# Attention and two MLPs on one core: pair 1's loads held back behind pair 0's k, v loaded by one queue, and softmax sums read out of PSUM ahead of two weight tiles

## What is computed

```python
batch, n_heads, seq, head_dim = (2, 12, 448, 64)
scores = scale * np.matmul(q, k.transpose(0, 1, 3, 2))
scores = cap * np.tanh(scores / cap)
scores = scores - np.max(scores, axis=-1, keepdims=True)
attn = np.exp(scores)
attn = attn / (np.sum(attn, axis=-1, keepdims=True) + 1e-09)
attn_out = np.matmul(attn, v)                 # 2 x 12 x 448 x 64
x = attn_out.transpose(0, 2, 1, 3).reshape(896, 768)
h = x @ w_in1                                 # 768 x 2048
x = np.maximum(h, 0.0) ** 2 @ w_out1          # 2048 x 768
h = x @ w_in2
out = h * (1.0 / (1.0 + np.exp(-h))) @ w_out2
```

## Time and profile before

| | us |
|---|---|
| median of 3 runs | 546.67 |
| lowest, highest | 546.26, 548.05 |
| the profiled execution, its time | 548.26 |
| the profiled execution, its span | 546.5 |
| PE busy in the span | 536.2 |
| DVE busy | 376.6 |
| ACT busy | 261.1 |
| POOL busy | 82.2 |

### The profile page before, as it was taken

How to read it: one execution, slowest core, us unless ns; L and a number is a source line. 1 busy time by engine, 2 the same in 40 slices (tenths; PEclk the granted TensorE clock), 3 DMA queues, 4 the chain that set the end, 5 groups by cost and what they waited for, 6 DMA issues and landing times.

```text
span 546.5 us, 7023 instructions
## 1 busy us (share of the span) xinstructions
PE 536.2 (98%) x2620; PEld 441.9 (81%) x2620; DVE 376.6 (69%) x597; ACT 261.1 (48%) x403; POOL 82.2 (15%) x54
## 2 busy tenths in 40 slices
PE   7999999999999999999999999999999999999996
PEld 5333333799999999999998999999999999999995
DVE  3199999877778552776789855556865345568985
ACT  3998998054444322445444434544533244454230
POOL 0899999300000000000000000000000000000000
PEclk9999999999999999999999999999999999999999
DMA  8885530151202202410211114102111241020646
GB/s 228 211 222 154 150 107 17 42 136 58 56 22 76 59 1 58 136 58 23 56 52 43 42 59 135 58 5 74 38 49 48 59 122 44 29 78 3 125 66 89
DMA packets 82117, 42.17 MB, mean 77 GB/s; under 512 B 26784, under 2 KB 79008, under 8 KB 82080
## 3 DMA queue, kind: packets, MB, share of 16 engines
q1 hardware_dynamic: 77664, 40.12, 28.0%
q10 hardware_dynamic: 4384, 1.57, 1.2%
q0 software_dynamic: 32, 0.00, 0.0%
HBM read 38.93 MB, written 2.75 MB: 76 GB/s over the span
## 4 chain that ended last, share of the span: by engine, by line
PE 80%; DVE 13%; issue 3%; ACT 1%; DMA 1%; ACTq 0%; DVEq 0%
PE banks L501 26%; PE banks L503 26%; PE banks L502 26%; DVE den L829 3%; PE banks L443 2%; DVE x_hi L838 1%; DVE rinv L833 1%; DMA qk_raw<-in_q_dram 1%; DVE att_o L836 1%; DVE den_r L826 1%; DVE w_hl L879 1%; DVE qk_f L814 1%; PE banks L432 1%; DVE qk_f L810 1%; DVE y L959 1%
## 5 line engine op out<-in xcount | busy, mean ns | idle before, releaser
L501 PE MATMUL banks<-x_hi,w_hl 128*128 128x448 f32 x384 | 140.7, 366 | 0.0
L503 PE MATMUL banks<-x_hi,w_hl 128*128 128x448 f32 x384 | 140.5, 366 | 0.0
L502 PE MATMUL banks<-x_lo,w_hl 128*128 128x448 f32 x384 | 140.5, 366 | 0.0
L501 PE MATMUL banks<-g_hi,w_hl 128*128 128x448 f32 x336 | 123.4, 367 | 0.2 <-DVE w_hl L879 0.2
L503 PE MATMUL banks<-g_hi,w_hl 128*128 128x448 f32 x336 | 123.2, 367 | 0.0
L502 PE MATMUL banks<-g_lo,w_hl 128*128 128x448 f32 x336 | 123.2, 367 | 0.0
L501 PEld LDWEIGHTS banks<-x_hi,w_hl 128*128 128x128 f32 x384 | 72.1, 188 | 7.6 <-issue 1.4
L503 PEld LDWEIGHTS banks<-x_hi,w_hl 128*128 128x128 f32 x384 | 72.1, 188 | 6.2
L502 PEld LDWEIGHTS banks<-x_lo,w_hl 128*128 128x128 f32 x384 | 72.1, 188 | 6.2
L874 DVE TENSOR_TENSOR w_hl<-w_raw,w_hl 128x768 fp32r<-128x768 f32 x32 | 32.5, 1016 | 57.5 <-ACT w_hl L650 57.4
L682 ACT ACTIVATE work<-banks 128x448 f32<-128x448 f32 x64 | 31.3, 541 | 78.2 <-PE banks L503 69.2
(11 more groups left out here) (64 smaller groups left out, 549.7 us busy)
## 6 DMA issues: line engine op xcount, KB each, us to landing
w_raw<-in_moe_w_in_dram SPq DMA_DIRECT2D x32, 384.0 KB, 3.4
w_raw<-in_moe_w_out_dram SPq DMA_DIRECT2D x24, 512.0 KB, 5.2
qk_raw<-in_k_dram SPq DMA_DIRECT2D x44, 112.0 KB, 2.5
qk_raw<-in_q_dram SPq DMA_DIRECT2D x44, 112.0 KB, 2.7
out_dram<-rows SPq DMA_DIRECT2D x40, 56.0 KB, 2.2
v_t<-in_v_dram SPq DMA_DIRECT2D x22, 96.0 KB, 2.7
qk_raw<-in_k_dram ACTq DMA_DIRECT2D x4, 112.0 KB, 4.2
qk_raw<-in_q_dram ACTq DMA_DIRECT2D x4, 112.0 KB, 5.7
```

Of the source, the lines that this page charges most:

```text
L501: pe.matmul(dst, hi[:, kk, :], mov_hi, start=start, stop=False, skip_group_check=onto)
L502: pe.matmul(dst, hi[:, kk, :], mov_lo, start=False, stop=False, skip_group_check=onto)
L503: return pe.matmul(dst, lo[:, kk, :], mov_hi, start=False, stop=stop, skip_group_check=onto)
```

## The change

In three parts. SP and ACT each wait, after their four DMAs of pair 0, until k of pair 0 has landed, and only then issue those of pair 1. All four v DMAs of the first two pairs are issued by SP, none by ACT. `finish` is cut in two: `take_sums` waits for PE's sums and transposes them out of PSUM, `finish` does the rest; in the slots the two follow each other as before, and at the hand-over `take_sums` comes ahead of the weight tile's low part.

```diff
-            def load_v(part, groups=range(C)):
+            def load_v(part):
 
                 first, last = V_PARTS[part], V_PARTS[part + 1]
-                for g in groups:
+                for g in range(C):
@@ SP
             load_head(0, 0, k_v, 0, s_first_in[0])
             load_head(0, 1, q_v, 0, s_first_in[1])
+            sp.wait_ge(s_first_in[0], 4 * DMA)
             load_head(1, 0, k_v, 0, s_qk_in[1])
             load_head(1, 1, q_v, 0, s_qk_in[1])
-            load_v(0, range(0, 2))
+            load_v(0)
             load_v_x(0)
@@ ACT
             load_head(0, 0, k_v, 1, s_first_in[0])
             load_head(0, 1, q_v, 1, s_first_in[1])
+            act.wait_ge(s_first_in[0], 4 * DMA)
             load_head(1, 0, k_v, 1, s_qk_in[1])
             load_head(1, 1, q_v, 1, s_qk_in[1])
-            for g in range(2, C):
-                at = g * CW * D
-                act.dma_start(v_t[BL * g:BL * g + BL, 0:2 * V_PARTS[1], :],
-                              v_main[:, 0:2 * V_PARTS[1], at:at + CW * D]).then_inc(s_v_in[0], DMA)
@@ DVE
-            def finish(j, den_bank):
+            def take_sums(j, den_bank):
 
                 dve.wait_ge(s_att, j.no + 1)
                 dve.transpose(den_r[:, :], den_bank).then_inc(s_den, 1)
+
+            def finish(j):
+
                 dve.wait_ge(s_den, 4 * j.no + 1)
@@ DVE, slot(j)
-                finish(j + -2, den_ps(j + -2))
+                take_sums(j + -2, den_ps(j + -2))
+                finish(j + -2)
@@ DVE, hand-over
-            tile_low(0, 0, 0)
-            finish(At(0, PAIRS - 3), den_ps(At(0, PAIRS - 3)))
-            tile_low(0, 0, 1)
-            for j in range(PAIRS - 2, PAIRS):
-                finish(At(0, j), den_ps(At(0, j)))
+            for j in range(PAIRS - 3, PAIRS):
+                take_sums(At(0, j), den_ps(At(0, j)))
+                if j < PAIRS - 1:
+                    tile_low(0, 0, j - (PAIRS - 3))
+                finish(At(0, j))
```

## The result

The changed kernel took 545.39 us (median of 6 runs, 545.13 to 545.6), the kernel before 547.19 us (6 runs, 546.26 to 548.63): a ratio of 0.9961 with a 95% interval of 0.9949 to 0.9973, so 1.5 to 2.8 us less. A second set, with other runs of the kernel before beside it, gave 0.9963 (0.995 to 0.9977). The forecast was 1.4 us less and 545.3 us. The gain is about 2 us or 0.4%, just over what a measurement of this kernel can tell from no change.

What follows compares the result with a forecast made beforehand. PE was taken as full from 104 us on, so only its earlier arrival saves time: 0.77 us at the start plus 0.63 us at the hand-over, 546.67 - 1.4 = 545.3 us, range 544.5 to 546.6.

Steps and rivals of the forecast that it cites:

- Where time can be saved: From 104 us on PE is full, so the change helps only by letting PE get there earlier.
- Change 2: Hand-over before the MLPs: transposing pair 9's sums before tile_low lets PE's next sums start 0.6 to 0.66 us earlier.
- an unbroken sequence starts 0.08 us before the modelled end: Hand-over: PE's sums of pair 10 would start at 93.48, its values ending at 93.56, 0.66 us earlier.
- The tight spot: Near 102 us, PE's product waiting for the second tile_low: only 0.15 us left after the release.
- rival 4: Hand-over: tile_low(1) holds PE up, or sums aren't the wait; gain there 0 to 0.3 us, chance 0.13.
- Change 1: Start: holding pair 1's loads until pair 0's k lands frees q, so PE's first scores come 0.77 us earlier.
- the upper bound: Start: if cap's DMA lands earlier too, first scores gain up to 1.0 us, limited by PE's warm-up.
- pair 1 costs nothing: Start: pair 1's delayed loads land at 8.8 to 10.7, transposed by 12.0 at the latest, the limit; no cost.
- What lands behind SP's queue: First 28 us: v and the loads of pairs 2 and 3, issued later on SP, still arrive in time; no cost.
- rivals 2 and 3: SP's queue late: PE stands 0.85 us at 19 us, 546.1, chance 0.10; v late: 547.6 us, chance 0.05.
- The sum: Whole kernel: 0.77 us at the start plus 0.63 us at the hand-over makes 1.4 us, all reaching the end.
- the front: The kernel's start up to PE's first scores and values: 0.77 us expected gain, bounds 0 and 1.0.

Runs made afterwards that it cites:

- late_wait: Changed kernel, but both queues hold pair 1's loads until q of pair 0, not k, has landed: 548.63 us, ratio 1.0020.
- the front alone: Kernel before with only the wait for k and v's loads on SP, old hand-over kept: 546.68 us, ratio 0.9985.
- the hand-over alone: Kernel before with only the new hand-over, sums taken out of PSUM first, loads as before: 546.14 us, ratio 0.9978.
- sp_waits: Changed kernel, but only SP waits for k; ACT issues its half of pair 1 at once: 546.70 us, ratio 0.9988.
- act_waits: Changed kernel, but only ACT waits for k; SP issues its half of pair 1 at once: 548.59 us, ratio 1.0005.
- half_wait_w10: Changed kernel, pair 1 held only until each queue's first k DMA has landed, 10 warm-up matmuls for 14: 545.36 us, ratio 0.9965.

## Why the prediction held, step by step

- **Where time can be saved.** Held. Behind the hand-over the two programs run alike but for about 1 us that comes and goes with the execution.
- **Change 2, 0.63 us.** The right mechanism, undersized by a quarter: 0.80 to 0.85 us. The term "an unbroken sequence starts 0.08 us before the modelled end" was too small: the sums start 0.75 us behind the last four values, so 0.17 us before their end at 0.92, which gives 0.76. The other 0.05 is in the sums themselves, after which the next matmul now comes at 0.85 and not 0.90 us. The tight spot (rival 4, 0.15 us) never came up: I had left tile_low at 1.89 us, and it took 1.33 and 1.32 in its new place (the last section says why), the second ending at 100.14 with PE at its product at 100.95.
- **Change 1, 0.77 us.** The right mechanism, too large by about 0.3 us: 0.98 us between the first two profiles, 0.5 on average over three pairs. q was freed: without the waits it was late again. cap's DMA came earlier too, as the upper bound had allowed, so PE's warm-up became the limit at the first scores, which came at 7.93 on average and not at 8.15. The step that failed is "pair 1 costs nothing". My last landing was 8.8 to 10.7 and the limit 12.0 for the transposes; they ended at 11.93 and 12.26 (turned from 10.76 and 11.09), so the slack I had counted on was not there. Its price was small: from first scores to first values it is 4.99 to 5.00 us in the three traces with the old loads and 5.08 to 5.20 in those with the new, 0.1 to 0.2 us. `late_wait` shows how near the edge is. The larger error was in the ground: the profiled execution before was 0.65 us slower at the start than the next one of the same program, and its first scores at 8.92 lie 0.37 us above the mean of the three old traces. So 0.77 + 0.22 - 0.37 - 0.14 makes the 0.5.
- **What lands behind SP's queue.** As worked out. v's last load was issued at about 8 and took 4.0 us (I took 3.5), pair 2's loads began at 10.49 (10.6) and were turned from 16.49 (16.55 to 17.85), pair 3's from 25.03 (24.6), with 26.2 for its end against scores at 26.62. None of them released PE, so rivals 2 and 3 did not come. Pair 3 has the least to spare, 0.3 us with the release and not the 0.9 that I had.
- **The sum.** By the traces' landmarks, with 0.5 for the front and 0.83 for the hand-over, it is 1.3 us, next to the forecast's 1.4. The runs say 1.8 and, against the larger set, 2.0 to 2.2, and their intervals reach down to 1.3 to 1.5. What lies between, if it is real, wasn't found; the front alone and the hand-over alone were measured at 0.8 and 1.2 us, each above its landmark by 0.3 to 0.4, with the landmark within its interval.
- **Where luck came in.** By the landmarks the two errors of size offset each other: the front 0.3 too much, the hand-over 0.2 too little. And that the forecast of 545.3 lies 0.1 from the measured 545.39 is luck too: it started from the median of three runs, 546.67, where 30 runs of the kernel before give 547.56, and that start was too low by about as much as the gain in the runs was larger than 1.4 us.
- **The chances.** I gave 0.25 to a gain over 0.3%, and 0.69 to none that can be told. The measured one is just over that line; with a sum 0.2 us below it, and a start uncertain by more than that, the split was too sure.

## What to carry to other kernels

A stall of PE on one reader of a PSUM bank was worth all of its length here, where PE is full on both sides of it (0.58 to 0.62 us of idle, 0.80 to 0.85 us gained), and the gain repeated to hundredths of a microsecond. Holding loads back to free an earlier one moves the bound to what was held back: ask by how much its own landing may slip, and what else is queued behind the wait on its engine (here a table load), before taking it as free. A microsecond between two profiles can be the execution's: here the landing of q, the length of PE's warm-up and the pace of the MLPs' matmuls all differed between executions of one program. A second profile of each program would have shown that the front's 1.0 us can't be read from one pair.

## What the runs showed of the hardware

- Matmuls of the MLPs came every 0.2027 or every 0.2067 us in stretches of up to 50 us, at a granted clock of 1.00 in both. Between 160 and 210 us it was 244 matmuls in one execution of a program and 248 in another. A stretch of 50 us is worth 1 us in 545. The time from ACT's first step in the MLPs to the end was 436.0 us in the two traces with two long slow stretches, 434.6 to 435.1 in the eleven with one, and 434.0 in `sp_waits`, with none. The cause is open.
- The 14 warm-up matmuls took 4.76 to 6.34 us, whatever the kernel: their rows start 0.21 us apart and from some point on 0.11 us, and that point lay at 5.1 us in one trace and hadn't come by 8.1 in another, the profile's granted clock being 1.00 throughout. The cause is open.
- DVE's split of a weight tile (128x768) took 1.89 us at 91.54 and 99.31 in the kernel before, 1.33 and 1.32 us at 91.04 and 98.82 in the changed one, and 0.95 us at 115.95, with POOL idle. POOL's instruction in flight ended 1.07 us after the start in both of the first (92.61 and 100.38), 0.51 us in both of the second (91.55 = 88.90 + 2.65, and 99.33). Each of the four ended 0.81 or 0.82 us behind the end of POOL's instruction, as though DVE had waited for it. DVE's next small step fits: the 128x14 one at 92.29 took 2.08 us, to 94.37, and 0.23 us with POOL idle; POOL's instruction beside it ended at 94.34. Instructions of DVE have to be priced by what POOL does in their new place, which I had not done. No run was made for it.
- PE's idle time of 2.48 us in `act_waits`, and of 0.91 and then 1.39 us in `late_wait`, was followed by a granted clock of 0.50 (1.2 GHz) for about 3 us. One of 1.05 us in the kernel before and of 0.97 us in `half_wait_w10`, each ahead of the first scores, was not.
